# Where the sums of the keys are taken, and when GpSimd starts on the weights, in an attention kernel that feeds two MLPs

## The reference

```python
batch, n_heads, seq, head_dim = (4, 8, 576, 64)
q_d = q.reshape(B, H, Sd, factor, D).mean(axis=3)      # factor = 4; k_d and v_d alike
out_d = sm_attn(q_d, k_d, v_d)                         # softmax(q k^T / sqrt(D)) v
out_up = np.repeat(out_d, factor, axis=2)
mask = np.abs(pos[:, None] - pos[None, :]) < factor
scores = np.where(mask, scale * q @ k^T, -1e9)
out_local = softmax(scores) @ v
x = (out_up + out_local)                               # 2304 tokens x 512
h = x @ w_in;  x = (np.maximum(h, 0.0) + alpha * np.minimum(h, 0.0)) @ w_out       # d_ff 2048
xn = x / rms * rms_g
return (silu(xn @ w_gate) * (xn @ w_val) @ w_out)                                # d_ff 1536
```

## Time and profile before

| | us |
|---|---|
| runs | 1014.29, 1013.84, 1010.44 (median 1013.84) |
| the profiled execution, device time | 1009.58 |
| its span | 1007.8 |
| PE busy | 986.0 (98%) |
| DVE busy | 528.3 (52%) |
| ACT busy | 407.0 (40%) |
| POOL busy | 113.4 (11%) |

### The profile page before, as it was taken

One profiled execution on the slowest core, in us unless ns is written; L12 is line 12 of the kernel. 1 busy time (PEld: TensorE's weight loads), 2 busy tenths in 40 slices (PEclk: granted clock), 3 DMA queues, 4 the chain that ended last, 5 costly groups with the idle time before them and its releaser, 6 DMA issues.

```text
span 1007.8 us, 19333 instructions
## 1 busy us (share of the span) xinstructions
PE 986.0 (98%) x7207; PEld 941.7 (93%) x7207; DVE 528.3 (52%) x961; ACT 407.0 (40%) x960; POOL 113.4 (11%) x122
## 2 busy tenths in 40 slices
PE   8899999999999999999999999999999999999998
PEld 7888999998999999999999999999999999999997
DVE  6887875765766758667456455234234234234211
ACT  6656544444444444444456344223223223223211
POOL 4665300002100012000011221000000000000000
PEclk9999999999999999999999999999999999999999
DMA  8931311013201032010154400100100100000000
GB/s 166 270 92 37 95 37 45 25 43 84 49 19 47 12 101 60 20 49 2 39 187 147 128 1 28 36 1 27 36 0 29 34 0 31 31 0 31 1 1 31
DMA packets 98801, 52.19 MB, mean 52 GB/s; under 512 B 60565, under 2 KB 92841, under 8 KB 98729
## 3 DMA queue, kind: packets, MB, share of 16 engines
q1 hardware_dynamic: 94584, 50.14, 17.8%
q10 hardware_dynamic: 4144, 1.03, 0.7%
HBM read 41.72 MB, written 9.44 MB: 51 GB/s over the span
## 4 chain that ended last, share of the span: by engine, by line
PE 88%; DVE 7%; issue 3%; ACT 2%; DVEq 0%; POOL 0%; POOLq 0%; ACTq 0%
PE banks L1266 30%; PE banks L1193 18%; PE banks L1179 17%; PE banks L1281 15%; PE banks L1160 2%; DVE pos L968 1%; PE banks L1144 1%; PE banks L1136 1%; PE banks L1122 1%; PE banks L1131 1%; PE banks L1165 1%; PE banks L1148 1%; ACT W_front L658 0%; PE banks L1229 0%; DVE g1lo L975 0%
## 5 line engine op out<-in xcount | busy, mean ns | idle before, releaser
L1266 PE MATMUL banks<-xnhi,W_front 128*128 128x384 f32 x672 | 176.0, 335 | 0.0
L1017 DVE TENSOR_TENSOR g<-banks,silu 128x384 f32<-128x384 f32 x72 | 40.1, 556 | 234.7 <-ACT silu L769 234.6
L1193 PE MATMUL banks<-g1hi,W_front 128*128 128x288 f32 x640 | 145.2, 303 | 0.0
L1179 PE MATMUL banks<-xhi,W_front 128*128 128x288 f32 x640 | 144.5, 303 | 0.0
L769 ACT ACTIVATE silu<-banks 128x384 f32<-128x384 f32 x72 | 35.4, 492 | 257.8 <-PE banks L1266 257.8
L1266 PEld LDWEIGHTS banks<-xnhi,W_front 128*128 128x128 f32 x672 | 121.9, 188 | 1.3
L968 DVE SCALAR_TENSOR_TENSOR pos<-neg,coef,pos 128x288 f32<-128x288 f32 x128 | 77.2, 603 | 80.3 <-ACT neg L726 80.2
L1266 PE MATMUL banks<-xnlo,W_front 128*128 128x384 f32 x336 | 112.4, 335 | 0.0
L1193 PEld LDWEIGHTS banks<-g1hi,W_front 128*128 128x128 f32 x640 | 107.2, 188 | 2.1
L1179 PEld LDWEIGHTS banks<-xhi,W_front 128*128 128x128 f32 x640 | 108.0, 190 | 0.7
L725 ACT ACTIVATE pos<-banks 128x288 f32<-128x288 f32 x128 | 52.2, 408 | 130.2 <-PE banks L1179 129.9
(11 more groups left out here) (156 smaller groups left out, 1903.7 us busy)
## 6 DMA issues: line engine op xcount, KB each, us to landing
W_raw<-in_moe_w_out_dram SPq DMA_DIRECT2D x26, 256.0 KB, 4.7
x_scratch<-xbuf SPq DMA_DIRECT2D x8, 576.0 KB, 3.6
xn<-x_scratch SPq DMA_DIRECT2D x6, 768.0 KB, 4.5
out_dram<-ysb SPq DMA_DIRECT2D x18, 256.0 KB, 2.1
vwin<-in_v_dram SPq DMA_DIRECT2D x90, 51.0 KB
W_raw<-in_moe_w_in_dram SPq DMA_DIRECT2D x16, 256.0 KB, 5.2
q_tok<-in_q_dram SPq DMA_DIRECT2D x56, 72.0 KB, 2.1
v<-in_v_dram SPq DMA_DIRECT2D x26, 144.0 KB
```

Source lines behind the costliest of these rows:

```text
L1017: dve.tensor_tensor(g2[:, c % 2, :], val_b[c % 2][:, 0:TB2], silu[:, c % 2, :], ALU.mult).then_inc(s_g2, 1)
L1179: last = pe.matmul(hb[c % 2][:, 0:TB1], w, x[:, t, :], start=(t + j == 0), stop=(t == KT - 1 and j == 2))
L1193: last = pe.matmul(acc[t][:, 0:TB1], w, g[:, c % 3, :], start=(c == 0 and j == 0), stop=(c == C1 - 1 and j == 2))
L1266: last = pe.matmul(bank[:, 0:TB2], w, x[:, t, :], start=(t + j == 0), stop=(t == KT - 1 and j == 2))
```

## The change

There are four edits.

- POOL no longer takes both parts of pieces 6, 8 and 10. Their high parts go to ACT and their low parts to POOL like the others. ACT copies the high part of piece 1 at the end of the first attention (H1), and SPLIT_IN_CHUNK has two pieces from chunk 0 on. SP loads the pieces in an order that fits this.
- POOL makes `ones` and the second half of the mask ahead of the sums of v, and starts on the weights when all four parts of the first x are split (s_xlo), no longer when the last probabilities are there (s_prob).
- DVE sums the queries (qd) at j = 0 of step A, where it did so with the last part of A.
- For batches 1 to 3 the sums of the keys (kd) go from one reduction on DVE to three additions on POOL, ahead of v_sums of the same pair. For batch 0 they stay on DVE.

```diff
-    EARLY, EARLY_POOL = (0, 2, 4), (6, 8, 10)
-    SPLIT_IN_CHUNK = [[n for n in (2 * c + 1, 2 * c + 6) if n < Q1 and n not in EARLY_POOL] for c in range(C1)]
+    EARLY = (0, 2, 4)
+    SPLIT_IN_CHUNK = [[n for n in (2 * c + 3, 2 * c + 6) if n < Q1] for c in range(C1)]
...
-    HI_ORDER = list(EARLY) + [n for chunk in SPLIT_IN_CHUNK for n in chunk] + LATE
+    HI_ORDER = list(EARLY) + [1] + [n for chunk in SPLIT_IN_CHUNK for n in chunk] + LATE
...
-    LO_POOL = list(EARLY_POOL) + [n for n in HI_ORDER if n not in LO_DVE]
+    LO_POOL = [n for n in HI_ORDER if n not in LO_DVE]
...
-    FIRST_ACT = "... D3 X2 X3 H4"
+    FIRST_ACT = "... D3 X2 X3 H4 H1"
...
-            for n in (4, 6, 8, 10, 1, 3):
+            for n in (4, 1, 3, 6, 5, 8):
                 load_piece(n)
             load_v(0, 1, 0)
-            for n in (5, 7, 12, 9):
+            for n in (10, 7, 12, 9):
                 load_piece(n)
...
             def piece_lo(n):
                 i = n if n < Q1 else n - Q1
-                if n in EARLY_POOL:
-                    wait_piece(pool, n)
-                    pool.tensor_copy(wpiece(i, 0), wraw(i)).then_inc(s_whi_pool, 1)
-                    pool.wait_ge(s_whi_pool, EARLY_POOL.index(n) + 1)
-                else:
-                    wait_hi(pool, n)
+                wait_hi(pool, n)
...
             mask_half(0)
+            pool.memset(ones[:, :], 1.0).then_inc(s_consts, 1)
+            mask_half(1)
             for p in range(G):
                 v_sums(0, p)
-            pool.memset(ones[:, :], 1.0).then_inc(s_consts, 1)
-            mask_half(1)
-
-            pool.wait_ge(s_prob, 2 * G)
+
+            pool.wait_ge(s_xlo, KT + BEGUN)
...
+            def k_sums(b, p):
+                m = G * b - G + p
+                drained(pool, b, 0, "A", p, FILLS[0] - 1)
+                src, dst = kT[:, p, :].rearrange("p (s r) -> p s r", r=FACTOR), kd[:, p, :]
+                pool.tensor_tensor(dst, src[:, :, 0], src[:, :, 1], ALU.add).then_inc(s_kd0, 1)
+                pool.wait_ge(s_kd0, 2 * m + 1)
+                pool.tensor_tensor(dst, dst, src[:, :, 2], ALU.add).then_inc(s_kd0, 1)
+                pool.wait_ge(s_kd0, 2 * m + 2)
+                pool.tensor_tensor(dst, dst, src[:, :, 3], ALU.add).then_inc(s_kd, 1)
+
             with pool.Fori(0, B - 1) as b:
                 for p in range(G):
+                    k_sums(b + 1, p)
                     v_sums(b + 1, p)
...
-                if kind == "A" and j == FILLS[h] - 1:
+
+                if kind == "A" and (j == 0 or j == FILLS[0] - 1 and is_first(b, h)):
                     drained(dve, b, h, kind, p, j)
-                    if h == 0:
+                    if j > 0:
                         dve.tensor_reduce(kd[:, p, :], kT[:, p, :].rearrange("p (s r) -> p s r", r=FACTOR),
                                           axis=AX.X, op=ALU.add).then_inc(s_kd, 1)
+                        return
                     dve.tensor_reduce(qd[:, p % 2, 0:SDH], qT[:, p % 2, :].rearrange("p (s r) -> p s r", r=FACTOR),
                                       axis=AX.X, op=ALU.add).then_inc(s_qd, 1)
```

More of the change, by code:

```diff
@@ L61, in attention_into_two_mlps_kernel @@
     W_FRONT, LOADS = 20, 16
-    EARLY, EARLY_POOL = (0, 2, 4), (6, 8, 10)
-    SPLIT_IN_CHUNK = [[n for n in (2 * c + 1, 2 * c + 6) if n < Q1 and n not in EARLY_POOL] for c in range(C1)]
+    EARLY = (0, 2, 4)
+    SPLIT_IN_CHUNK = [[n for n in (2 * c + 3, 2 * c + 6) if n < Q1] for c in range(C1)]
     LATE = list(range(Q1, Q1 + Q2))
-    HI_ORDER = list(EARLY) + [n for chunk in SPLIT_IN_CHUNK for n in chunk] + LATE
+    HI_ORDER = list(EARLY) + [1] + [n for chunk in SPLIT_IN_CHUNK for n in chunk] + LATE
     LO_DVE = list(EARLY) + [n for n in LATE if n % 2 == 0]
-    LO_POOL = list(EARLY_POOL) + [n for n in HI_ORDER if n not in LO_DVE]
+    LO_POOL = [n for n in HI_ORDER if n not in LO_DVE]
     FILLS = (3, 1)
     FIRST_PE = "W8 A0 W2 A1 W2 B0 W2 A2 W3 B1 A3 W6 B2 K0 W1 C0 W1 B3 W4 D0 W8 C1 W3 C2 D1 W1 C3 D2 D3"
-    FIRST_ACT = "A0 A1 A2 P0 E0 A3 P1 E1 C0 H0 P2 E2 D0 P3 E3 C1 X0 K0 C2 H2 D1 C3 D2 X1 D3 X2 X3 H4"
+    FIRST_ACT = "A0 A1 A2 P0 E0 A3 P1 E1 C0 H0 P2 E2 D0 P3 E3 C1 X0 K0 C2 H2 D1 C3 D2 X1 D3 X2 X3 H4 H1"
     FIRST_DVE = "A0 A1 B0 A2 B1 F0 A3 B2 B3 F1 D0 F2 F3 X0 L0 D1 L2 X1 D2 D3 X2 X3 L4"
@@ L209, in attention_into_two_mlps_kernel @@
         s_whi = sem("s_whi")
-        s_whi_pool = sem("s_whi_pool")
         s_wlo = [sem("s_wlo_dve"), sem("s_wlo_pool")]
@@ L222, in attention_into_two_mlps_kernel @@
         s_kd = sem("s_kd")
+        s_kd0 = sem("s_kd0")
         s_qd = sem("s_qd")
```

## The result

The changed kernel takes 1017.85 us (median of 7 runs, 1016.78 to 1018.89). The kernel before, run beside it, takes 1010.75 (median of 7, 1009.48 to 1014.29). The ratio is 1.0062, with a 95% interval of 1.0043 to 1.0080, so the change costs 6 to 7 us. The forecast was 1015.0, with 1009 to 1021 as its range. The absolute time lies inside, but the loss is about twice the 3.0 us of the sum, and it is over the 0.5% that a measurement can tell, where 0.15 had been given. The profiled execution took 1017.85 us, 8.3 more than the one of before, which lay 1.2 under the median of the kernel before; so the profiles show about 1 us more than the medians do.

A forecast was written before the change was run, and what follows sets the result against it. TensorE, busy 986.0 of 1007.8 us, was taken as the bound, its remaining waits ended by DVE. The terms +0.5, +3.0 and -0.5 gave +3.0 us on a mean of 1012.0, so 1015.0 us, range 1009 to 1021.

The forecast's parts named there:

- three signs of being wrong: Key additions over 0.8 us, waits at the other nine B, or idling from 35 to 60 us shrinking over 1.5 us.
- TensorE starts 0.9 us earlier: Start of the first MLP: DVE's subtractions, free of POOL, let TensorE start 0.9 us earlier, bounds 0 and 1.0.
- The clock's 1.6 us: Behind the first MLP's start: 1.6 us may return if TensorE's clock stays up; counted at nothing in the likeliest case.
- I take 1.4: Chunks 0 to 2 of the first MLP: POOL's new pairs of weights hold DVE 1.4 us, of 0 to 3.1.
- +0.5: At the first C of the first MLP: DVE 1.4 later, start 0.9 earlier, together +0.5 us, bounds -1.6 and +2.2.
- +1.0 us for each of the three B: First B of batches 1 to 3: POOL's key additions make each 1.0 us later, +3.0 together, bounds 0 and +6.0.
- -0.5: Other B, C and D of batches 1 to 3: 0.5 of the 0.70 at 137.78 comes back, bounds -0.7 and +3.
- The start wins: Rival: the earlier start stays and waits of 0.67 and 0.70 go, about -1.4 us, 1010.6 us; chance 0.18.
- Slower by far: Rival: POOL's strided key additions make all twelve B of batches 1 to 3 wait, about +14 us, 1026 us; chance 0.12.
- third rival: The first edit does nothing, the 1.88 us gap at the start stays: about +4 us, 1016 us; chance 0.08.

The follow-up runs named there:

- queries_first: The kernel before with the queries summed at j = 0 of step A and all keys left on DVE: 1008.63 us, ratio 0.9978.
- keys_only: The kernel before with only the keys' part: POOL sums the keys of batches 1 to 3, queries summed ahead: 1014.64 us, ratio 1.0040.
- keys_behind_v: The keys' part alone on the kernel before, but with POOL's sums of v ahead of those of the keys: 1011.49 us, ratio 1.0008.
- queries_spread: The kernel before with queries summed ahead and the first of two high parts in a chunk copied behind ACT's neg: 1006.88 us, ratio 0.9958.
- keys_pair0_dve: The keys' part alone on the kernel before, but with the keys of pair 0 left on DVE: 1012.88 us, ratio 1.0013.
- fill_gap: The kernel before with 16 useless multiplications on TensorE in front of the first MLP: 1012.72 us, ratio 1.0026.
- weights_only: The changed kernel with the keys' sums on POOL and the early sum of queries taken back: 1014.69 us, ratio 1.0037 against the kernel before.
- weights_spread: The weights' part alone, with the first of two high parts in a chunk copied behind ACT's neg: 1011.69 us, ratio 1.0000 against the kernel before.
- no_lo_six: The weights' part alone, with POOL copying raw weights instead of subtracting for six pieces' low parts: 1011.79 us, ratio 1.0004 against the kernel before.
- all_spread: The change's weights with high parts spread behind ACT's neg, queries summed ahead, all keys on DVE: 1008.78 us, ratio 0.9980 against the kernel before.

## Why the prediction fell short

That 1017.85 lies in the range of 1009 to 1021 is in part luck. The forecast was added to a mean of 1012.0, and beside the changed kernel the kernel before took 1010.75: the base was 1.3 us too high, and the change of +3.0 was 4.1 too low. Nor did any of the three signs of being wrong appear (an addition of keys over 0.8 us, waits at the other nine B of batches 1 to 3, less idling from 35 to 60 us), since none looked at the C of the later batches or at the clock behind the first C.

**"TensorE starts 0.9 us earlier."** The mechanism held: DVE's subtractions took 0.68, and the gap is 0.92. In the profiled execution the last step of the first attention stood at 33.09, 0.72 later than before (32.37), so that of the 0.96 only 0.23 is seen in the start itself (34.98 against 35.21). The size came from a gap of 1.88 that is not typical. In the five later profiles with the weights as in the kernel before and no fillers (queries_first, keys_only, keys_behind_v, queries_spread, keys_pair0_dve) the gap was 1.11, 1.35, 1.35, 1.36 and 0.93, the last with the clock at 0.50 ahead of it. With the weights of the change it was 0.92 in all five profiles. Against the first five the gain is 0 to 0.4. What the term missed is DVE's third subtraction, at 36.53, which was relieved of 1.08 us behind the start.

**The clock's 1.6 us, counted "at nothing".** It came back in the start. That it is eaten at 54.84 was right for two thirds, by fill_gap (1.09 of 1.57). What I left out is the other side: a TensorE that comes earlier to a DVE that comes later idles 3.5 us, and there the clock falls. In the profiled execution that cost 1.0 net at the first C and 1.6 behind the third. This term was not in the sum; with the nine waits at C below, as large, it is the largest of those missed. It isn't the same in every execution, as the clocks of weights_only show (0.990 to 0.997).

**"I take 1.4" for POOL's pairs, "+0.5" with the start.** The two holds came to 1.8 us, so this size was nearly right. Two things failed. The bounds took the earlier start and DVE's delay as one difference at one C, +2.2 at most; the weights alone cost 3.7 (2.3 to 5.1). And ACT's high parts were called "one more in front of each relu" but priced at nothing: once DVE was held, ACT was the next in the chain, and its second high part cost 0.5 more.

**"+1.0 us for each of the three B."** It was +0.84, +0.84 and +0.60, 2.3 us in all where I took 3.0. The forecast waits of 1.2 to 2.0 are 1.37 to 1.42; POOL ends two of them, and for the third no releaser is named. The additions took 0.47, 0.56 and 0.65 us.

**"-0.5" for the other B, C and D.** Here the sign was wrong. The 0.70 at 137.78 went, but that isn't shown to be the edit's doing: it is absent in weights_only too, where DVE has all the sums, and in fill_gap such a wait stands at 272.33 (0.68). Nine waits at C came, 2.6 us. The step had named the cause, "v_sums of a pair now stands behind k_sums, and falls on F", and had put it only into the bound of +3. keys_behind_v shows it: with the order turned they are gone, and so are 3 of the 4 us. The loads of v and of the pieces cost nothing, as said: no idle time of TensorE in the MLPs is ended by a DMA that wasn't before.

**The rivals.** "The start wins" fell, since the clock did stay up and the kernel got slower all the same. "Slower by far" fell too: the longest addition is 0.66 us, under the 0.78 from which the other B would wait, and none of them does. The Trainium skill has VectorE at a lower rate on a source that hops at every element (Vector Engine (DVE) Microarchitecture Reference, section Measured stream behaviour on trn2); on POOL the first addition, with both inputs at a stride of four words, took 0.48 us in the median (0.47 to 0.55), against the 0.49 of the contiguous fit, so GpSimd shows no such loss here. The third rival's 1016 lies nearest to the result, for a reason that isn't true: its gap of 1.88 did not stay.

The sum again with the runs' numbers: weights +3.7, keys +4.0, together 7.7, against 6 to 7 measured. The forecast had +0.5 and +2.5: it was too low by about 3 us in the first term (the clock, ACT's high parts) and by 1.5 in the second (the waits at C).

## What to carry over

Where two engines meet, the change of each has to be followed up to the meeting: an earlier comer and a later partner add to one wait, and an idle time of several microseconds on TensorE can cost its clock too, there and not where the edit is. When a helper's work is moved to a free engine, check what that engine's next task now falls on; here the order of two calls was worth about 3 us. And an idle time that one execution shows should be read in a second one before it is spent in a sum.

## What the runs showed that I had not expected

- The clock doesn't follow the idle time in front of it alone. Behind 1.82 us at the third C it stayed at 1.00 in the kernel before and fell to 0.62 over 85.5 to 90 us in the changed one. Behind 1.35 us at the start it was 0.62 over 34.5 to 39 us in keys_only, and behind 1.36 it was 1.00 in queries_spread. At the first C it fell behind 3.06 in weights_spread and, with less idling, behind 2.12 in no_lo_six (0.61 over 57 to 60 us), and stayed at 1.00 behind 3.05 in all_spread. So one profile doesn't tell whether a given idle time costs the clock.
- POOL and DVE hold each other. POOL's third addition of v took 1.17 us beside the division, 0.72 alone. Four low parts in a row took 6.25 us where twice two would be 5.0.
- A copy of 512 elements on POOL took 0.59 us in no_lo_six, a subtraction of as many 1.25.
- 16 fillers of TensorE at the start took 3.84 us and delayed the MLP by 1.74: they did not fit into the gap that they were to fill.
